# Rows of the first two expert tiles picked by token before the scatters of the routing

## What is computed

```python
x = attention(q, k, v).transpose(0, 2, 1, 3).reshape(2304, 512)   # blocks of 64, softmax
# experts
skip_score = x @ w_skip
do_compute = skip_score > 0
out = x.copy()
xc = x[do_compute]
logits = xc @ w_gate                      # 8 experts
e_idx = np.argmax(logits, axis=1)
gate_w = softmax(logits)[np.arange(len(xc)), e_idx]
for e in range(8):
    mask = e_idx == e
    h = np.maximum(xc[mask] @ w1[e], 0.0)         # w1: 512 x 1024
    y[mask] = gate_w[mask, None] * (h @ w2[e])    # w2: 1024 x 512
out[do_compute] = xc + y
# dense layer
h = out @ w_in                            # 512 x 2048
g = np.maximum(h, 0.0) + alpha * np.minimum(h, 0.0)
return g @ w_out                          # 2048 x 512
```

## Time and profile before

| | us |
|---|---|
| median of 3 runs | 910.12 (907.75 to 910.98) |
| the profiled execution | 910.3 |
| its span | 908.4 |
| TensorE busy | 822.5 (91%) |
| VectorE busy | 435.7 (48%) |
| ScalarE busy | 265.2 (29%) |
| POOL busy | 238.0 (26%) |

### The profile page before, as it was taken

One profiled execution on the slowest core, in us unless ns is written; L12 is line 12 of the kernel. 1 busy time (PEld: TensorE's weight loads), 2 busy tenths in 40 slices (PEclk: granted clock), 3 DMA queues, 4 the chain that ended last, 5 costly groups with the idle time before them and its releaser, 6 DMA issues.

```text
span 908.4 us, 15588 instructions
## 1 busy us (share of the span) xinstructions
PE 822.5 (91%) x5243; PEld 724.0 (80%) x5244; DVE 435.7 (48%) x894; ACT 265.2 (29%) x643; POOL 238.0 (26%) x193
## 2 busy tenths in 40 slices
PE   6799999999703989999968999999999999999997
PEld 5588888888503979999857988998998998898986
DVE  3476776777741333323364554444354344443442
ACT  4466656656321212212311112112112112112111
POOL 6224244432053681230547861001001001000000
PEclk9899999999955999999997999999999999999999
DMA  6388888574166846613834312002002002000001
GB/s 127 75 237 211 228 230 207 145 174 112 37 228 236 301 185 208 229 48 127 311 141 116 91 35 70 0 0 69 0 0 69 0 0 69 0 0 35 1 1 35
DMA packets 95972, 99.66 MB, mean 110 GB/s; under 512 B 64336, under 2 KB 64336, under 8 KB 95440
## 3 DMA queue, kind: packets, MB, share of 16 engines
q1 hardware_dynamic: 87136, 70.79, 27.3%
q0 software_dynamic: 4448, 15.73, 5.5%
q10 hardware_dynamic: 4368, 12.88, 3.9%
HBM read 64.78 MB, written 24.12 MB: 98 GB/s over the span
## 4 chain that ended last, share of the span: by engine, by line
PE 75%; SPq 6%; POOL 5%; DMA 5%; issue 4%; DVE 3%; ACT 2%; DVEq 0%; ACTq 0%; POOLq 0%
PE bank L836 22%; PE bank L847 22%; PE bank L786 7%; PE bank L800 7%; PE bank L685 4%; PE bank L696 3%; PE bank L673 3%; POOL x_slots L555 2%; PE bank L719 2%; PE bank L649 2%; SPq L364 2%; PE bank L667 1%; SPq L388 1%; DMA stage<-in_moe_w_in_dram 1%; POOL wi_lo L568 1%
## 5 line engine op out<-in xcount | busy, mean ns | idle before, releaser
L1287 DVE TENSOR_SCALAR g_sb<-bank,alpha_sb 128x384 f32<-128x384 f32 x96 | 59.3, 618 | 218.8 <-PE bank L836 218.6
L1005 ACT CAST g_hi<-g_sb 128x384 fp32r<-128x384 f32 x96 | 49.4, 515 | 322.0 <-DVE g_sb L1289 322.0
L836 PE MATMUL bank<-u_hi,wi_hi 128*128 128x384 f32 x384 | 130.5, 340 | 1.4 <-DVE u_lo L1260 1.4
L836 PE MATMUL bank<-u_hi,wi_lo 128*128 128x384 f32 x384 | 130.4, 340 | 0.0
L836 PE MATMUL bank<-u_lo,wi_hi 128*128 128x384 f32 x384 | 130.0, 339 | 0.0
L847 PE MATMUL bank<-wo_lo,g_hi 128*128 128x512 f32 x288 | 113.8, 395 | 0.0
L847 PE MATMUL bank<-wo_hi,g_hi 128*128 128x512 f32 x288 | 112.8, 392 | 0.8 <-DVE g_lo L1293 0.8
L847 PE MATMUL bank<-wo_hi,g_lo 128*128 128x512 f32 x288 | 113.5, 394 | 0.0
L786 PEld LDWEIGHTS bank<-rows_t,w_sb 128*128 128x128 f32 x832 | 96.5, 195 | 2.6 <-DVE rows_t L1208 1.5
L786 PE MATMUL bank<-rows_t,w_sb 128*128 128x128 f32 x832 | 96.8, 278 | 1.1 <-DVE rows_t L1208 1.1
L892 ACT ACTIVATE p_sb<-bank,neg_max 128x128 f32<-128x128 f32 (+2 forms) x144 | 79.2, 552 | 56.2 <-DVE neg_max L1034 53.7
(11 more groups left out here) (152 smaller groups left out, 1283.4 us busy)
## 6 DMA issues: line engine op xcount, KB each, us to landing
w_sb<-in_moe_w_dram ACTq DMA_DIRECT2D x6, 2048.0 KB, 7.8
w_sb<-in_moe_w_dram SPq DMA_DIRECT2D x6, 2048.0 KB, 8.7
q_t<-q_t SPq DMA_DIRECT2D x64, 160.0 KB, 2.5
w_sb<-in_moe_w_dram SPq DMA_DIRECT2D x16, 512.0 KB, 6.5
x_slots<-zeros SPq DMA_DIRECT2D x14, 512.0 KB, 3.6
v_nat<-in_v_dram SPq DMA_DIRECT2D x32, 128.0 KB, 2.4
y_out<-in_moe_w_out_dram POOLq DMA_DIRECT2D x16, 256.0 KB, 2.9
out_dram<-y_out SPq DMA_DIRECT2D x16, 256.0 KB, 2.7
```

Source lines behind the costliest of these rows:

```text
L836: last = pe.matmul(dst, w[:, j, P * f:P * f + P], u[:, j, :], start=z == 0, stop=z == len(terms) - 1)
L1005: act.copy(g_hi[:, f % GB, :], g_sb[:, f % 2, :]).then_inc(g_hi_done, 1)
L1287: dve.tensor_scalar(g, a, 0.0, alpha_sb[:, f:f + 1], ALU.min, ALU.mult).then_inc(neg_done, 1)
```

## The change

x is written to HBM once more during attention, as a table `x_all` of tokens by 512. `save_rows` does it on SP's queue, a batch at a time: after `load_step(5)`, after `load_step(9)`, after `load_step(13)`, and in two pieces at the end. To that end `load_step(1)` is moved ahead of the loops, and each load of a quarter of w1 and w2 comes one step later.

After `slot_i`, VectorE, TensorE and VectorE find which tokens stand in the 256 slots of tiles 0 and 1: `at_row` compares each token's row within its tile with 0 to 127 (three pieces of 128 x 768), `id_at_tile` holds the token's number where its tile is 0 or 1, 18 matmuls of 4 columns add them up, and the result is `token_i`. `counting` and `ids` are tables of numbers made by two matmuls and two copies of ScalarE ahead of that. POOL gathers the rows of tiles 0 and 1 from `x_all` with two indirect DMAs, waits for the first to land, and only then issues the 18 scatters. Its wait for `rows_loaded` behind the scatters is gone. SP no longer fetches tiles 0 and 1; it waits for both gathers, sets `rows_loaded` to 32, and then zeroes `y_slots` and waits for the scatters as before, ahead of fetching tile 2. VectorE splits w2 of expert 1 after the copy of tile 0's rows instead of before, and its gate steps come after `token_i`.

```diff
+            def save_rows(b, pairs):
+                lo, hi = P * pairs[0], P * pairs[1]
+                sp.wait_ge(x_done, 2 * (HP * b + pairs[1]))
+                sp.dma_start(x_all.rearrange("(t p) d -> p t d", p=P)[:, b * FULL:(b + 1) * FULL, lo:hi],
+                             x_tok[:, b * FULL:(b + 1) * FULL, lo:hi]).then_inc(x_saved, 16)
+                tail = B * MAIN + TAIL * b
+                sp.dma_start(x_all[tail:tail + TAIL, lo:hi], x_tail[:, b, lo:hi]).then_inc(x_saved, 16)
...
             sp.wait_ge(zeros_set, 1)
+            load_step(1)
             for par in range(2):
                 with sp.Fori(1, KD + 1) as m:
-                    load_step(m + KD * par)
+                    load_step(m + 1 + KD * par)
...
+                save_rows(par, (0, HP))
-            with sp.Fori(2 * KD + 1, PAIRS - 2) as n:
+            with sp.Fori(2 * KD + 2, PAIRS - 2) as n:
                 load_step(n)
-            load_step(PAIRS - 2)
+            save_rows(2, (0, HP))
+            load_step(PAIRS - 2, False)
             sp.wait_ge(pv_done, 2 * (PAIRS - 1))
             load_v(PAIRS - 1)
+            save_rows(B - 1, (0, HP - 1))
+            save_rows(B - 1, (HP - 1, HP))
...
+            for g in range(DIRECT):
+                sp.wait_ge(rows_picked[g], 16)
+            sp.sem_inc(rows_loaded, 16 * DIRECT)
             with sp.Fori(used, SLOT_TILES) as g:
                 sp.dma_start(y_slots[bass.ds(g * P, P), :], zeros[:]).then_inc(y_zeroed, 16)
             sp.wait_ge(scattered, 16 * T_TILES)
-            sp.wait_ge(zeros_dma, ZEROED)
-            load_rows(0)
-            sp.wait_ge(rows_loaded, 16)
-            load_rows(1)
...
             pool.wait_ge(zeros_dma, ZEROED)
+            pool.wait_ge(x_saved, 16 * 2 * (B + 1))
+            pool.wait_ge(token_ready, 1)
+            for g in range(DIRECT):
+                pool.indirect_dma_start(out=rows_in[:, g, :], out_offset=None, in_=x_all[:, :],
+                                        in_offset=bass.IndirectOffsetOnAxis(ap=token_i[:, g:g + 1], axis=0)
+                                        ).then_inc(rows_picked[g], 16)
+            pool.wait_ge(rows_picked[0], 16)
             for t in range(T_TILES):
...
-            pool.wait_ge(rows_loaded, 32)
...
+            for z, (lo, hi) in enumerate(PIECES):
+                pe.wait_ge(picks_ready, z + 1)
+                for t in range(lo, hi):
+                    last = pe.matmul(NUMBERS, at_row[:, t, :], id_at_tile[:, t].rearrange("p a g -> p (a g)"),
+                                     start=t == 0, stop=t == T_TILES - 1)
+            last.then_inc(tokens_done, 1)
...
+            for lo, hi in PIECES:
+                part = [P, hi - lo, P]
+                dve.tensor_tensor(at_row[:, lo:hi], counting[:].unsqueeze(1).to_broadcast(part),
+                                  row_i[:, lo:hi].unsqueeze(2).to_broadcast(part), ALU.is_equal).then_inc(picks_ready, 1)
+            dve.wait_ge(tokens_done, 1)
+            step(dve.reduce_sum(token_f[:], NUMBERS.rearrange("p (a g) -> p g a", a=2), AX.X))
+            dve.tensor_copy(token_i[:], token_f[:]).then_inc(token_ready, 1)
```

More of the change, by code:

```diff
@@ L55, in program @@
     SKIPPED = B * S + E * P
+    DIRECT = 2
     q_h = q.rearrange("b h s d -> (b h) s d")
@@ L86, in __call__ @@
                 return t
+        x_all = nc.dram_tensor("x_all", (B * S, D), F32, kind="Internal").ap()
         START = (nc.sbuf_base + 63) // 64 * 64
@@ L98, in program @@
         slot_i = sb("slot_i", [P, T_TILES], U32)
+        token_i = sb("token_i", [P, DIRECT], U32)
         from_i = sb("from_i", [P, T_TILES], U32)
@@ L175, in program @@
         from_f = sb("from_f", [P, T_TILES], F32)
+        token_f = sb("token_f", [P, DIRECT], F32)
+        row_i = sb("row_i", [P, T_TILES], U32)
+        slot_tile_i = sb("slot_tile_i", [P, T_TILES], U32)
+        counting = sb("counting", [P, P], BF16)
+        ids = sb("ids", [P, T_TILES, 2], BF16)
         rows_in = sb("rows_in", [P, 2, D], F32)
@@ L181, in program @@
         y_sb = sb("y_sb", [P, 2, D], F32)
+        picks = Region(REST, REST + half)
+        at_row = picks("at_row", [P, T_TILES, P], BF16)
+        at_tile = picks("at_tile", [P, T_TILES, DIRECT], BF16)
+        id_at_tile = picks("id_at_tile", [P, T_TILES, 2, DIRECT], BF16)
         stage = sb("stage", [P, 1, FD], F32)
@@ L194, in program @@
         zeros_dma = sem("zeros_dma")
+        x_saved = sem("x_saved")
+        counting_done = sem("counting_done")
+        counting_ready = sem("counting_ready")
+        picks_ready = sem("picks_ready")
+        tokens_done = sem("tokens_done")
+        token_ready = sem("token_ready")
+        rows_picked = [sem(f"rows_picked{g}") for g in range(DIRECT)]
         y_zeroed = sem("y_zeroed")
@@ L307, in program @@
         COUNTS = bank[5][:, 0:E + 1]
+        COUNTING, NUMBERS = bank[3], bank[4][:, 0:2 * DIRECT]
+        PIECES = [(z * T_TILES // 3, (z + 1) * T_TILES // 3) for z in range(3)]
         HIDDEN = [bank[0], bank[1], bank[2], bank[5]]
@@ L388, in swap, with load_step @@
                         sp.dma_start(dst.bitcast(F32), src.bitcast(F32)).then_inc(swapped[h], 16)
-            def load_step(n):
-                if not isinstance(n, int):
+            def load_step(n, more=True):
+                if more:
                     sp.wait_ge(split_done, n + 1)
@@ L755, in _ @@
             to_rows(PAIRS - 1)
+            pe.wait_ge(router_const, 4)
+            pe.matmul(COUNTING[:, 0:P], ones_b[:], before[:], start=True, stop=True)
+            pe.matmul(COUNTING[:, P:P + 1], before[:], ones_b[:, 0:1], start=True, stop=True).then_inc(counting_done, 1)
             pe.wait_ge(member_ready, 1)
-            pe.wait_ge(router_const, 4)
             flat = member_b[:].rearrange("p t e -> p (t e)")
@@ L935, in _ @@
             last.then_inc(logits_tails, 1)
+            act.wait_ge(counting_done, 1)
+            act.copy(counting[:], COUNTING[:, 0:P])
+            act.copy(ids[:, :, 1], COUNTING[:, P:P + 1].to_broadcast([P, T_TILES])).then_inc(counting_ready, 1)
             act.wait_ge(x_done, 2 * PAIRS)
@@ L967, in _ @@
             act.wait_ge(routed, 1)
-            rows_copy(0)
+            act.wait_ge(rows_picked[0], 16)
+            act.copy(rows[:], rows_in[:, 0, :]).then_inc(rows_copied, 1)
             def second_hi(par, n):
@@ L1176, in _ @@
             dve.tensor_copy(member_b[:], member[:]).then_inc(member_ready, 1)
+            dve.wait_ge(counting_ready, 1)
+            step(dve.tensor_scalar(ids[:, :, 0], counting[:, 0:T_TILES], float(P), None, ALU.mult))
             dve.wait_ge(ranks_done, 1)
@@ L1191, in _ @@
             step(dve.reduce_sum(slot_f[:], place[:], AX.X))
-            dve.tensor_copy(slot_i[:], slot_f[:]).then_inc(routed, 1)
+            step(dve.tensor_copy(slot_i[:], slot_f[:]))
+            dve.sem_inc(routed, 1)
+            step(dve.tensor_scalar(row_i[:], slot_i[:], P - 1, None, ALU.bitwise_and))
+            step(dve.tensor_scalar(slot_tile_i[:], slot_i[:], P.bit_length() - 1, None, ALU.logical_shift_right))
+            all_s = [P, T_TILES, DIRECT]
+            step(dve.tensor_tensor(at_tile[:], counting[:, 0:DIRECT].unsqueeze(1).to_broadcast(all_s),
+                                   slot_tile_i[:].unsqueeze(2).to_broadcast(all_s), ALU.is_equal))
+            all_s = [P, T_TILES, 2, DIRECT]
+            step(dve.tensor_tensor(id_at_tile[:], at_tile[:].unsqueeze(2).to_broadcast(all_s),
+                                   ids[:].unsqueeze(3).to_broadcast(all_s), ALU.mult))
+            for lo, hi in PIECES:
[5 more added lines that the diff above has]
+            dve.tensor_copy(token_i[:], token_f[:]).then_inc(token_ready, 1)
             dve.wait_ge(exp_done, 1)
@@ L1224, in tiles, with first_lo @@
                     dve.tensor_copy(parity(y_sb, g), RESULT[:]).then_inc(y_evac, 1)
-            for e in range(2):
+            def first_lo(e):
                 dve.wait_ge(w2_hi_done, e + 1)
@@ L1229, in _ @@
                 dve.tensor_tensor(lo, raw, hi.bitcast(F32), ALU.subtract).then_inc(w2_split, 1)
-            dve.wait_ge(routed, 1)
+            first_lo(0)
             dve.sem_inc(y_evac, 1)
@@ L1233, in _ @@
             rows_out(0)
+            first_lo(1)
             with dve.Fori(0, E // 2) as e2:
```

## The result

| | before | after |
|---|---|---|
| median, runs side by side | 910.01 (907.75 to 910.98, 4 runs) | 929.5 (928.09 to 932.03, 4 runs) |
| the profiled execution | 910.3 | 928.1 |
| its span | 908.4 | 926.3 |

The ratio is 1.0212 (95% interval 1.0186 to 1.0237): 19.5 us slower, where 7.4 were forecast. The sign was right. The size was not, and 929.5 lies outside the range.

What follows compares the result with a forecast made beforehand. The prediction took POOL's chain of loads and splits before tile 2, not tile 0's start, as the bound on the experts' part. 910.3 + 6.2 for the saves + 1.2 for the expert part gave 917.7 us, range 910 to 922.

Steps and rivals of the forecast that it cites:

- The sign: Whole kernel: slower, above 914.8 us, was given chance 0.62; the same 0.32 and faster 0.06.
- What bounds the kernel: Routing to experts: POOL's 39.72 us of work before tile 2 stays; tile 0's earlier start gains at most 3.82 us.
- Part 3: Attention: saves after steps 5 and 9 delay SP's q and k loads, 3.1 us each, +6.2 us together.
- a clock sentence for tile 2: Tile 2's second product: TensorE's clock is low after the longer wait, but was before too; no difference taken.
- Part 1 and 2: From slot_i to tile 2: picks, gather and what the scatters then lie beside make tile 2 1.2 us later.
- scatters slowed: Scatters on POOL: one more is slow beside VectorE's w_lo, +0.9 us, with 0 to 1.9 as ends.
- the two stage loads: POOL's loads behind the scatters: the first loses its quiet place, the second may gain; 0, from -1.7 to +3 us.
- part of -0.9: POOL's splits before tile 2: expert 2's w_lo escapes VectorE's w_lo, which may hit wi_lo instead; half of 1.85 us gained.
- The rule on ports: Scatters on POOL: by a skill page VectorE's tensor_tensor slows none, which would make the sum 0.9 us lower.
- (a): Attention: saves disappear in DMA's idle share, 2 x 1.0 us at most; 911 to 914.5 us, chance 0.25.
- (b): Expert part: POOL's chain gets shorter by 5.6 us, faster than before; 904.7 to 906.7 us, chance 0.08.
- (c): More contention: saves 3.6 to 4.5 us each, stage loads +3, scatters +1.9; 921.5 to 926 us, chance 0.09.

Runs made afterwards that it cites:

- the two reordered kernels: POOL splits expert 2's first half of w2 between the two quarters of w_in: in the light-saves kernel 908.71 us, in the kernel before 903.34 us.
- the kernel with saves only: The kernel before with load_step(1) ahead of the loops and all saves at the changed kernel's places, no picks or gathers: 922.44 us, ratio 1.0155.
- The half and the double save: The kernel with saves only, its save behind step 5 cut to 0.52 MB and that behind step 9 doubled to 2.10 MB, no tails: 921.84 us, one execution.
- light-saves kernel: The changed kernel with the saves of batches 0 to 2 moved behind steps 11, 12 and 13, where no weights are loaded: 920.61 us, ratio 1.0128.
- zeros late: The light-saves kernel with SP's zeroing of unused y_slots tiles moved behind the loop over experts 0 to 5: 919.3 us, ratio 1.0104.
- weights first and zeros late: The light-saves kernel with expert 2's first half of w2 split between the w_in quarters and y_slots zeroed behind experts 0 to 5: 908.91 us, ratio 0.9991.
- shift alone: The kernel before with load_step(1) ahead of the loops, each weight load one step later, nothing else: 909.88 us over ten runs, ratio 1.0017.

## Why the prediction was wrong in size

**What bounds the kernel: right.** TensorE's wait for POOL's w_lo grew from 3.82 to 15.59 (forecast 15 to 20), and the two reordered kernels confirm POOL's chain as the limit by experiment: taking a stage out of it gave 11.9 us with the picks. One bound was too low. Without the picks the reordering gave 7.1 us in the medians (4.6 to 8.9 by the interval), where TensorE's wait of 3.82 was to be all there was. In the profiled run, the longest of the seven, tile 2 came 3.4 sooner; where the others won the rest no trace shows.

**Part 3, the saves: the step that failed.** Two saves at 3.1 were to give +6.2. The pairs cost 5.4 to 6.2 us each (19.6 to 19.9 against 13.7 to 14.3), and attention +11.0 in the kernel with saves only and +14.0 in the kernel after. The term was mis-sized in two ways.

First, the delay of the transfers was 4.0 us of wait, not 3.1. The rate of the busiest window, 383 GB/s, was the wrong price. Here are the windows of after, around the first save and on an undisturbed step (stretch, length, busy us by engine, granted clock, DMA share, GB/s):

```profile
100.00:114.00 14.00, 11.85 (x106) 9.36 (x104) 9.10 (x25) 8.45 (x24) 1.50 (x1) 1.00 0.90 259
114.00:121.00 7.00, 5.08 (x23) 4.99 (x24) 1.45 (x3) 0.46 (x2) 5.01 (x4) 0.53 0.86 215
128.00:142.00 14.00, 13.91 (x125) 11.67 (x124) 10.28 (x28) 9.09 (x28) 5.04 (x4) 1.00 0.78 207
```

The engines were busy to 0.90 and moved 259 GB/s. The row with 383 was another mix of transfers. At 259 GB/s 1.18 MB are 4.6 us; the measured slope of 2.18 us a MB is 459 GB/s, so neither rate prices a save alone, and the constant of 1.4 us is part of it. The weights' own price, 3.6 for the like amount, which the prediction worked out and passed over for 3.1, was nearer.

Second, the clock. The prediction had a clock sentence for tile 2 and none for attention. In the window behind the wait the granted clock is 0.53, near the lower of the two levels (1.2 of 2.4 GHz), after a pair at 1.00; from the end of the wait at 115.92 to 120.50 alone it is 0.50. The ten matmuls of L764 took 2.64 us there, and 1.41 at the same place before. From the end of the wait to the product with v (L741) TensorE works without a pause, and took 6.51 and 6.24 us in the two pairs of the kernel after, 5.57 and 5.64 with saves only, against 4.01 in the kernel before: the clock costs 1.6 to 2.5 us a save. Before the clock fell TensorE had idled 3.98 us, where it waited 0.17 in the kernel before. The half and the double save show the same behind waits of 2.55 and 5.99: 5.59 and 6.92 us.

**The mechanism of part 3 was half right.** The waits of TensorE for q_t stand at the forecast pairs, and light steps take the saves for almost nothing, as the argument from the earlier trace rows would have it. But the reason given, SP's queue in which saves stand ahead of loads, falls with the saves on POOL's queue. Shifting the weights cost 0, as said. The kernel after loses 3.1 us more in attention than the one with saves only. Some 1.5 of them are its longer stretches at the lower clock; the rest lies mostly in the second and third pair (14.79 and 14.31 against 13.72 and 13.88), where no save stands, and is not explained.

**Part 1 and 2: right in kind, +6.1 instead of +1.2.** Term by term:

| term | forecast | measured |
|---|---|---|
| scatters start later (from slot_i) | 8.44 | 9.40 |
| wait for fetched tiles gone | -7.25 | -7.55 |
| scatters slowed | +0.9 | +1.0 |
| the two stage loads | 0 (-1.7 to +3) | +1.67, +1.69 |
| first wi_hi | part of -0.9 | +1.99 |
| w_lo | part of -0.9 | -1.95 |
| small differences | 0 | -0.2 |
| sum | 1.2 | 6.1 |

VectorE's and TensorE's small steps were well priced: the comparisons took 2.69 for three (forecast 2.9). The gather landed in 3.96 rather than 3.3, and POOL took up its issue 0.9 us after token_i rather than 0.3. The stage loads are the term that failed, just beyond its own upper bound of 3: 3.4 together. The removed wait had given the scatters time to drain before the first load; that this came back as length of the load is shown in the light-saves kernel (zeros late: 5.97 instead of 8.70) and carried over to the kernel after. For the second, experts' weights are the likely cause, but no run isolates it. One premise did not come true: w1 of expert 2 was to be asked for 20 us earlier, and it was 4.1, counted from slot_i (last section). The trade of w_lo against wi_hi came out even; VectorE's step (timeline) hit the whole of one and left the other alone:

```profile
308.89 2.28 DVE L1319 TENSOR_TENSOR w_lo<-w_sb,w_hi 128x2048 fp32r<-128x2048 f32 x1
```

POOL's wi_hi, which began at 309.05 beside it, took 5.59 for 3.60 at the second quarter. "I take no difference" for the clock at tile 2 left out 0.7: its 24 products took 8.13 against 7.39, and the next tile's 5.62 against 5.61.

**The rule on ports.** The prediction weighed a page of the Trainium skill, SBUF — State Buffer, "Who interferes with whom", by which VectorE's tensor_tensor would slow no scatter. The trace disagrees: two scatters took 2.83 and 1.90 us against 0.97 for nearly all others, and two w_lo of VectorE (278.64 and 280.84, 2.28 and 2.29 long) lie beside them. So does the issue of the second gather, with a w_lo of VectorE at 272.70:

```profile
273.51 2.30 POOL L594 DMA_INDIRECT rows_in<-x_all,token_i  x1 [0.30 <-issue]
```

Not all time of VectorE does this; it was the big w_lo each time, and not every time, as the scatter at 258.21 of the earlier trace rows took 0.97 beside one. These are coincidences in the timelines, but they repeat: in each of the five other kernels with picks one late scatter took 2.11 to 3.07 us, and a w_lo of VectorE lies beside it, at another time in each (283.27 with w_lo at 283.21 with light saves, 287.53 with w_lo at 286.82 with weights first and zeros late). No run was made to move w_lo away.

**The rivals.** (a), saves that vanish, falls: it would need pairs of 14 us. It is what happens with the saves in light steps, though. (b) falls with the expert part. (c), more contention, is in kind the case that came, at chance 0.09: stage loads +3.4 against its +3, saves beyond its 3.6 to 4.5. It too had no term for the clock and so ended at 926.

**Do the parts add up?** In medians the saves alone cost 13.7 and the light-saves kernel 11.9, both against 908.75, 25.6 together against 19.5. Of the excess 2.5 us can be seen: the expert part was 80.95 in the one and 78.48 after. The rest lies within the intervals of the three ratios, each some 2 to 4 us either way.

## What to carry to other kernels

Price an added transfer where it will lie, not by the best rate elsewhere: look for the step that can take it up, here one without weights, with 3.6 us of slack ahead of the swap, and put it there. Another queue bought nothing here. The zeros are the warning: moved out of one tight place they cost about as much in the next. To the wait that a transfer causes on TensorE add the stretch at the lower clock behind it, here 1.6 to 2.5 us for 4. And before making an early step earlier, find the last wait of the stretch; here the order of POOL's own work was worth 7 us with a dozen lines, and the picks with their saves cost 5.4 on top of it.

## What the hardware showed that was not expected

The issue of a load on SP's queue stretches while a save is under way, whichever queue the save stands in: the last k load's issue from 1.02 us (shift alone) to 2.40 with the save on POOL's queue, the last q load's from 0.70 to 3.11 with the save on SP's, and the first two q loads' from 1.25 to 2.92 on a light step.

In the profiled execution of the kernel after, ScalarE stood twice between two steps of tile 0 (timeline, columns as above), for something the profile calls remote:

```profile
291.40 0.39 ACT L1016 ACTIVATE h_hi<-bank 128x256 fp32r<-128x256 f32 x1 [5.10 <-remote]
...
304.23 0.38 ACT L1016 ACTIVATE h_hi<-bank 128x256 fp32r<-128x256 f32 x1 [12.45 <-remote]
```

These steps start 1.8 to 2.8 us apart in the kernels with light saves and with saves on POOL's queue. It pushed the request for w1 of expert 2 to 304.51, and may have hidden or made part of the stage loads' length. It is not what made the expert part longer, though: without such a stop it was 80.95 (light saves, stage loads 8.70 and 9.31) and 82.83 (saves on POOL's queue, 9.85 and 9.51), and TensorE waits there for the rows of tile 2 instead (13.12 and 13.45). The kernel after had some luck in its 78.48. What ScalarE waited for stays open.
